# Moving parts of the next batch between v's tiles: o's second half one tile earlier, mean squares and k'v one tile earlier, both k'v copies on ScalarE

## The reference

```python
kv = einsum('bhsd,bhde', k, v)                    # 8 heads of 64: k'v is 64 x 64
o = q @ kv
x = o / sqrt(mean(o*o, -1) + 1e-6) * g_norm       # heads side by side: 576 x 512
h = relu(x @ w_in); u, v = h[:, :512], h[:, 512:]
v_n = (v - mean(v)) / sqrt(var(v) + 1e-6)         # over the 512 columns
gated = u * (w_spatial @ v_n + b_spatial)
y = gated @ w_out
h2 = relu(y @ w_in2)                              # 576 x 1024
out = (h2 * sigmoid(conv3(h2))) @ w_out2          # conv3 along the rows
```

## Time and profile before

| | |
|---|---|
| median of 3 runs | 788.32 us (788.27 to 788.42) |
| profiled execution | 788.02 us, of which the span is 786.2 us |
| TensorE busy | 780.0 us, 99% of the span |
| VectorE busy | 583.1 us, 74% |
| ScalarE busy | 422.0 us, 54% |
| granted TensorE clock | 0.999 of full speed |

### The profile page before, as it was taken

The page is one execution under the profiler, slowest core; times in us unless marked ns, Lnnn a source line. Parts: engine busy times, 40 slices in busy tenths (PEclk is TensorE's granted clock), DMA queues, the critical chain, the costliest instruction groups (busy, mean ns, idle before and its releaser), DMA issues.

```text
span 786.2 us, 15138 instructions
## 1 busy us (share of the span) xinstructions
PE 780.0 (99%) x5654; PEld 702.3 (89%) x5654; DVE 583.1 (74%) x1262; ACT 422.0 (54%) x753; POOL 29.5 (4%) x40
## 2 busy tenths in 40 slices
PE   9999999999999999999999999999999999999997
PEld 7679899897988979899999898998989899898986
DVE  3765875866477484757899899497986979689791
ACT  4664452635335263432457757375774747567562
POOL 4342000000000000000000000000000000000000
PEclk9999999999999999999999999999999999999999
DMA  9872738575261642222092202231021212102102
GB/s 327 306 254 63 270 96 302 179 246 208 61 225 61 195 150 61 107 59 107 8 360 90 107 24 105 68 106 54 20 108 46 105 53 105 54 14 105 54 0 67
DMA packets 35005, 96.92 MB, mean 123 GB/s; under 512 B 2738, under 2 KB 9106, under 8 KB 30228
## 3 DMA queue, kind: packets, MB, share of 16 engines
q1 hardware_dynamic: 33476, 90.09, 33.7%
q10 hardware_dynamic: 1488, 6.30, 2.1%
HBM read 66.11 MB, written 30.28 MB: 123 GB/s over the span
## 4 chain that ended last, share of the span: by engine, by line
PE 96%; DMA 1%; DVE 1%; ACT 1%; SPq 1%; issue 0%; ACTq 0%; DVEq 0%
PE ps L458 28%; PE ps L643 25%; PE ps L635 21%; PE ps L484 11%; PE ps L427 2%; PE ps L411 2%; PE ps L491 2%; PE ps L562 1%; DMA work<-w_out_T_dram 1%; PE ps L437 1%; DVE h_and_sums L1286 0%; DVE t_then_s L1186 0%; PE ps L550 0%; SPq L279 0%; PE ps L450 0%
## 5 line engine op out<-in xcount | busy, mean ns | idle before, releaser
L643 PE MATMUL ps<-w_in_split,v_hg_split 128*128 128x512 f32 x832 | 194.9, 389 | 0.0
L643 PEld LDWEIGHTS ps<-w_in_split,v_hg_split 128*128 128x128 f32 x832 | 155.7, 188 | 32.3
L458 PE MATMUL ps<-w_sp_split,v_hg_split 128*128 128x288 f32 x896 | 120.1, 295 | 0.0
L458 PEld LDWEIGHTS ps<-w_sp_split,v_hg_split 128*128 128x128 f32 x896 | 119.3, 188 | 0.0
L458 PE MATMUL ps<-x_operand_split,w_in_split 128*128 128x288 f32 x768 | 103.8, 295 | 0.0
L458 PEld LDWEIGHTS ps<-x_operand_split,w_in_split 128*128 128x128 f32 x768 | 102.1, 188 | 0.7 <-issue 0.2
L484 PE MATMUL ps<-w_in_split,x_operand_split 128*128 128x512 f32 x384 | 92.0, 392 | 0.0
L484 PEld LDWEIGHTS ps<-w_in_split,x_operand_split 128*128 128x128 f32 x384 | 71.1, 188 | 17.3 <-issue 3.1
L1137 DVE TENSOR_TENSOR work<-ps,work 128x576 f32<-128x576 f32 x32 | 24.1, 756 | 68.8 <-PE ps L458 68.6
L1286 DVE TENSOR_TENSOR h_and_sums<-h_and_sums,ps 128x288 f32<-128x288 f32 x160 | 68.5, 450 | 7.7 <-PE ps L635 7.2
L1286 DVE TENSOR_TENSOR h_and_sums<-work,ps 128x288 f32<-128x288 f32 x64 | 28.2, 450 | 46.8 <-PE ps L635 46.3
(11 more groups left out here) (124 smaller groups left out, 1068.4 us busy)
## 6 DMA issues: line engine op xcount, KB each, us to landing
kv_raw<-kv_main_dram SPq DMA_DIRECT2D x8, 2048.0 KB, 9.8
q_raw<-q_T_dram SPq DMA_DIRECT2D x8, 1152.0 KB, 5.1
operand_scratch<-t_then_s SPq DMA_DIRECT2D x8, 1152.0 KB, 4.7
operand_raw<-operand_scratch SPq DMA_DIRECT2D x8, 1152.0 KB, 5.7
sq_then_r<-r_scratch SPq DMA_DIRECT2D x14, 576.0 KB, 7.0
operand_scratch<-work SPq DMA_DIRECT2D x24, 288.0 KB, 2.7
operand_more_raw<-operand_scratch SPq DMA_DIRECT2D x8, 864.0 KB, 7.3
w_out_split_scratch<-v_hg_split ACTq DMA_DIRECT2D x2, 2048.0 KB, 8.6
```

The lines of the kernel that those rows point to most:

```text
L458: last = pe.matmul(pair[bank][:, c, :], st, mo[:, c * HALF:(c + 1) * HALF], start=(n == 0), stop=(n == len(steps) - 1))
L643: last = pe.matmul(PS[:, ROW_BANK[i], :], x, wout2[:, w, F_ORDER[e], :], start=(e == 0 and n == 0), stop=(e == FT - 1 and n == len(PASSES) ...
```

## The change

The change rewrites the order in which each engine's `body` issues its steps.

- `V_TILES` becomes 0, 1, rest, 2, 3.
- TensorE: o's pairs 2 and 3 follow v's tile 1 and not tile 2; the sums of squares and k'v follow tile 2, ahead of tile 3. Three waits that stand at the last matmul of a tile move with them.
- ScalarE: `o_copy` and `square` of pairs 2 and 3 are at p = 1 and not p = 2. At p = 4, `v_hi` of p = 3 stands ahead of `v_relu`. `root` is at p = 3, followed by `kv_copy`, which now writes both halves (four copies).
- VectorE: at p = 4, `v_lo` of p = 3 stands ahead of `v_stats`. `mean_square` and `inverse_root` are at p = 3. It no longer calls `kv_copy` for batch b+2.

```diff
-V_TILES = [0, 1, 2, FULL, 3]
+V_TILES = [0, 1, FULL, 2, 3]
...
# TensorE, v_product: waits at the last matmul of tile i
-                        if i == 2:
+                        if i == 1:
                             pe.wait_ge(s_xr, b + 1)
                             pe.wait_ge(s_vr, b * NT + 1)
                         if ahead:
                             if i == 0:
                                 o_ready(b + 1, 1)
+                            if i == 1:
+                                o_ready(b + 1, 3)
                             if i == 2:
-                                o_ready(b + 1, 3)
-                            if i == 3:
                                 square_ready(b + 1)
...
# TensorE, body
                     v_product(b, i, ahead)
-                    if ahead and i in (0, 2):
-                        o_product(b + 1, i)
-                        o_product(b + 1, i + 1)
-                if ahead:
-                    square_sum(b + 1)
-                if two_ahead:
-                    kv_product(b + 2)
+                    if ahead and i in (0, 1):
+                        o_product(b + 1, 2 * i)
+                        o_product(b + 1, 2 * i + 1)
+                    if ahead and i == 2:
+                        square_sum(b + 1)
+                    if two_ahead and i == 2:
+                        kv_product(b + 2)
...
# ScalarE, kv_copy
-                for half in (0, 1):
-                    last = act.activation(kvd[half * D:(half + 1) * D, :, 0, :],
-                                          PS[0:D, KV_BANK, 0:MT * D].rearrange("p (m e) -> p m e", m=MT), ACT.Copy)
-                last.then_inc(s_kvd0, 1)
+                for c, done in ((0, s_kvd0), (1, s_kvd1)) if both else ((0, s_kvd0),):
+                    for half in (0, 1):
+                        last = act.activation(kvd[half * D:(half + 1) * D, :, c, :],
+                                              PS[c * D:(c + 1) * D, KV_BANK, 0:MT * D].rearrange("p (m e) -> p m e", m=MT), ACT.Copy)
+                    last.then_inc(done, 1)
...
# ScalarE, body
                 for i in range(NT):
+                    if i == NT - 1:
+                        v_hi(b, i - 1)
                     v_relu(b, i)
-                    if ahead and i in (0, 2):
-                        o_copy(b + 1, i)
-                        square(b + 1, i)
-                    if i:
+                    if ahead and i in (0, 1):
+                        o_copy(b + 1, 2 * i)
+                        square(b + 1, 2 * i)
+                    if 0 < i < NT - 1:
                         v_hi(b, i - 1)
...
-                    if ahead and i == NT - 1:
+                    v_root(b, i)
+                    if ahead and i in (0, 1):
+                        o_copy(b + 1, 2 * i + 1)
+                        square(b + 1, 2 * i + 1)
+                    if ahead and i == 3:
                         root(b + 1)
-                    v_root(b, i)
-                    if ahead and i in (0, 2):
-                        o_copy(b + 1, i + 1)
-                        square(b + 1, i + 1)
+                    if two_ahead and i == 3:
+                        kv_copy(b + 2, True)
...
# VectorE, body
                 for i in range(NT):
+                    if i == NT - 1:
+                        v_lo(b, i - 1)
                     v_stats(b, i)
-                    if ahead and i == NT - 1:
+                    if ahead and i == 3:
                         mean_square(b + 1)
-                    if i:
+                    if 0 < i < NT - 1:
                         v_lo(b, i - 1)
                     v_normalise(b, i)
-                if two_ahead:
-                    kv_copy(b + 2)
-                if ahead:
-                    inverse_root(b + 1)
+                    if ahead and i == 3:
+                        inverse_root(b + 1)
```

More of the change, by code:

```diff
@@ L496, in u_product @@
                 if m == 1:
-                    pe.wait_ge(s_vr, b * NT + 4)
+                    pe.wait_ge(s_vr, b * NT + 3)
                 elif m == 2:
@@ L678, in _, with kv_copy @@
         def _(act):
-            def kv_copy(a):
+            def kv_copy(a, both=False):
                 act.wait_ge(s_kv, a + 1)
                 act.wait_ge(s_o, a * MT)
-                for half in (0, 1):
-                    last = act.activation(kvd[half * D:(half + 1) * D, :, 0, :],
-                                          PS[0:D, KV_BANK, 0:MT * D].rearrange("p (m e) -> p m e", m=MT), ACT.Copy)
-                last.then_inc(s_kvd0, 1)
+                for c, done in ((0, s_kvd0), (1, s_kvd1)) if both else ((0, s_kvd0),):
[3 more added lines that the diff above has]
+                    last.then_inc(done, 1)
             def o_copy(a, m):
```

## The result

The changed kernel takes 790.26 us (median of 9 runs, 789.7 to 791.2), the kernel before 788.32 us beside it (787.83 to 788.65). The ratio is 1.0024, with a 95% interval of 1.0015 to 1.0033. It is slower by 1.94 us. The forecast was 789.5 us and a range of 788.1 to 790.7. The result lies inside that range, but above the band of 789.0 to 790.0 us that the prediction gave its main account, and inside the 790.0 to 791.0 us of its rival in body 0.

What follows compares the result with a forecast made beforehand. TensorE's own work, the start and its waits were taken to bound the kernel. Matmuls 0.0, moved waits 0.0 and last body +1.15 us, added to 788.32, gave 789.5 us, range 788.1 to 790.7.

Steps and rivals of the forecast that it cites:

- main account: The forecast itself for the whole kernel: 789.0 to 790.0 us, chance 0.63.
- What bounds the kernel: Whole kernel: TensorE's own work, the start and its waits; TensorE busy 780.0 of 786.2 us.
- The last body: Last body: fourth tile's split and subtraction now precede the fifth tile's Relu and statistics; VectorE's first combined weight +1.15 us.
- All three places where TensorE should wait: Third spatial product 0.3 us, phase two's third product 0.3, VectorE's sums about 0.55 more; parts of the one 1.15.
- nothing shows: Rival: the last body's delay is swallowed before phase two's sums or overlaps keep it short; 788.3 us, chance 0.17.
- The matmuls: TensorE's switches between kinds of matmul, seven bodies: 0.0 us, at most 0.7 either way.
- The waits that move: Bodies 0 to 6: moved copies, squares, splits and loads stay in time for TensorE; 0.0 us, to +0.3.
- the second o copy: Bodies: needed at tile 1's last matmul, in time by 0.4 us; rival that it is late, chance 0.09.
- the squares: Bodies: needed by TensorE at tile 2's last matmul, claimed in time by 1.4 us.
- comes out within 0.1 us of where it was: A body's last `v_lo` hardly moves, standing behind u's second product in ScalarE's order before and after.
- Body 0 collides with GpSimd: Rival: held VectorE operations delay body 0's last `v_lo` past its 1.5 us of slack; 790.0 to 791.0 us, chance 0.07.
- sign of being wrong: Combined weight starts at 388 us yet TensorE waits no longer, or a body's length moves by over 0.1 us.

Runs made afterwards that it cites:

- e1: Changed kernel with the old order of the fifth tile's split and subtraction put back in the last body alone; 789.2 us, ratio 1.0005 to the kernel before.
- e2: Kernel before, with the fourth tile's split and subtraction ahead of the fifth tile's Relu and statistics in the last body alone; 789.64 us beside 788.48.
- e8: Changed kernel with squares and k'v behind v's last tile again, on TensorE alone; 790.14 us in one execution.
- e6: Changed kernel with inverse_root of body 0 alone put back behind the last tile; 790.12 us, ratio 1.0017 to the kernel before.
- e9: Changed kernel with the second half of the doubled k'v copied by VectorE again; 790.89 us in one execution.
- e5: Kernel before, with phase two's 16 border columns set by GpSimd instead of VectorE; 787.45 us beside 788.48.
- e7b: Changed kernel with the last body's order put back, body 0's inverse_root behind the last tile and its q load behind k and v; 789.69 us, ratio 1.0016.

## Why the prediction was right, and where it was short

**What bounds the kernel** held: TensorE is at 99% on both sides, and every difference is a wait of TensorE or a switch.

**The last body** held: +1.15 us to the first combined weight, as forecast to the hundredth, and 1.11 at the end. e1 takes it away, e2 brings it by itself (+1.38 with the rest tile as the fourth). All three places where TensorE should wait were found, with 0.44, 0.32 and 0.32 us for the forecast 0.3, 0.3 and 0.55. The rival "nothing shows" is refuted by e1 and e2.

**The matmuls**, put at 0.0 within 0.7 us in seven bodies, measured +0.04 each, together 0.22 us in bodies 1 to 6 (e8 shows it for bodies 1 to 5 and body 6), and the same 0.04 inside body 0's 0.53 (e6). Taking "k'v to v for k'v to u" as an even exchange was a little off: what u gains does not quite pay for what the tile behind k'v costs more.

**The waits that move**: the second o copy and the squares made TensorE wait in no body, so the narrowest slack, 0.4 us, was enough. (The copy ended 5.87 to 5.94 us into bodies 1 to 5 and 6.15 us into body 6, where the prediction has it asked for at 6.2 to 6.4.) The copies of k'v are free in bodies 1 to 5 (e9).

**The step that failed** is the sentence that the last `v_lo` of a body "comes out within 0.1 us of where it was", and for body 0 that "I count the same end after the change". It holds in bodies 1 to 5, within 0.04 us. In body 6 it is wrong too: the last subtraction ended 26.35 us into the body and not 25.19, 1.16 later, much as in the last body; body 6 has no k'v between its tiles either, which is the likely reason and was not tested. It cost TensorE nothing, for the spatial product starts only 29.5 us in.

In body 0 it came 1.8 us later, overran its 1.5 us, and the body grew by 0.53 us (47.43 for 46.90), of which e6 gives back 0.49. This is the rival "Body 0 collides with GpSimd" in its mildest size: it priced two more holds at 0.5 us of overrun, and gave itself 0.07. e6 shows the path: r ahead of the last tile's statistics, with ScalarE's remaining splits and the last split of v behind them. I had named the GpSimd holds, and left out that they would now fall on VectorE steps for which ScalarE's queue waits.

No run takes the holds away and leaves the order. The rows allow an estimate: between the rest tile's subtraction and the last one VectorE lost about 3.0 us to holds in the changed kernel and 2.3 in e6, and stood waiting for ScalarE 1.97 and 0.97 us. So of the 1.5 us between these two kernels some 0.6 is more time held and some 1.0 more waiting.

The Trainium skill (SBUF — State Buffer, "SBUF: two separate sides") has VectorE and GpSimd under an exclusive lock on a shared port pair. The row at 64.83 agrees: 1.59 us for an operation of 0.31 us, which started 0.01 us behind the GpSimd operation and ended 0.16 us behind its end. By that rule the change could cost time in body 0, and it did.

**Sum.** Forecast 1.15 + 0 + 0; measured 1.11 + 0.53 + 0.22 = 1.86 us in the stretches and 1.94 in the medians. So the prediction was right in its range, its direction and its main mechanism, and 0.8 us short in size. Its own sign of being wrong, a body's length that moves by over 0.1 us, was met in body 0. The slowdown of 0.24% is also over its mark of 0.2%, to which it had given 0.21 against 0.75 for no clear change. The range held because its upper edge was drawn to take in this rival at its mildest.

## What to carry to other kernels

Two engines that hand a tile back and forth are bound by the length of the round, and it matters which steps stand inside the other engine's waits: one split and subtraction put ahead of the next tile's Relu and statistics cost 1.15 us where the round was the bound, and nothing in the bodies where the matmul engine had other work, even in body 6, where the same steps came 1.16 us later. Look for a change's cost in the first and last turns of a loop, where part of the work that hides it is missing or foreign work is added. And before moving large steps, follow the line from the last stop of the busiest engine backwards: sixteen tiny memsets held two engines there and were worth 0.8 us.

## What the runs showed of the hardware

- A stop of TensorE costs more than the idle time beside it. Before the change the row at 420.63 shows 0.34 us, but that product starts 1.30 us behind the one before it, where 0.80 is usual, and what follows is slower too: from that product to the last layer's first matmuls 428.81 - 420.63 = 8.18 us, where e5, without the stop, has 428.63 - 420.63 = 8.00. I did not find out why.
- VectorE operations with two SBUF inputs that started beside a GpSimd operation were held, the longest of them to 1.2 to 1.6 us, for 0.2 to 0.8 us otherwise. A RECIPROCAL, with one input, took 1.05 us beside GpSimd (e6, 66.40) and 1.04 alone (changed kernel, 62.80).
- The first body began between 40.28 us (before) and 41.65 us (e7b) in the profiled executions, of kernels that do not differ up to there. This alone spreads the whole time by over a microsecond, more than most of the effects studied.
